# An attention output laid out as 96r + 32k + p instead of 3p + k, in a kernel of linear attention and two feed-forward stages

## The chip, the cores and the metric

The kernel runs on one core of one Trainium2 chip. The metric is the device time of one execution in microseconds, as the median of several runs. The profile shows one execution of its own. All arithmetic that matters here is float32 on TensorE, where one product of float32 operands appears in the trace as two MATMUL instructions (called passes below), each with its own LDWEIGHTS.

## The reference

```python
for t in range(S):                       # B, H, S, D = 4, 8, 768, 48
    state = f[:, :, t, :, None] * state + einsum('bhd,bhe->bhde', k[:, :, t], v[:, :, t])
    y[:, :, t] = einsum('bhd,bhde->bhe', q[:, :, t], state)      # f = sigmoid(f_logit)
x = y.transpose(0, 2, 1, 3).reshape(B * S, H * D)                # 3072 x 384
h = x @ w_in                                                     # 384 x 2048
x = (h * sigmoid(1.702 * h)) @ w_out                             # 2048 x 384
p = domain_probs / (domain_probs.sum(-1) + 1e-9)                 # 4 experts
out = sum over e of p[:, e] * (relu(x @ w1[e]) @ w2[e])          # w1: 384 x 1024
```

## The kernel before

The work falls into eight halves of a batch entry (384 tokens each: `HALVES`), each in three chunks (`CH`) of 128 tokens. The eight heads are held as four pairs (`PAIRS`), the two heads of a pair in the two 64-partition halves. Attention of a chunk is a masked score matrix (built level by level, `level`), its product with v, plus the product of the running state with q.

The program has four stretches. First the attention of half 0 alone (0 to 60 us). Then, seven times over, the attention of half n beside the first feed-forward of half n-1 (60 to 540 us): `both` goes through 18 slots, and in each slot TensorE does `hidden` (nine matmuls of 384 columns with w_in for one block of 128 hidden units), then the attention steps that the table `plan` puts there, then `layer_out` (nine matmuls with w_out, two slots behind). Then the first feed-forward of half 7, then the experts up to the end. I call the attention halves beside a feed-forward half 1 to half 7.

The attention output of chunk c is step `y`. In `plan`, y of chunk 0 (y0) stands in slot 13, y1 in slot 15, y2 in slot 16, each followed by step `update` of the state where one is wanted: TensorE multiplies v with k (L1781), VectorE adds the result to the faded state (L1406). y2 needs the state of update 1: its first matmul already waits for it, since it writes the PSUM bank that update 1 is read from.

From half 1 on, `y_columns` writes y straight in the layout that w_in wants: features on partitions, tokens on columns, as three tiles m of 128 features. A column tile of TensorE (32 output rows, `tile_position=(0, 32r)`) belongs to pair r. Feature dm stands in tile m at partition p with dm = 3p + m, so the 32 rows of pair r in tile m are every third of its 96 features: 16 of the one head, 16 of the other. For each m there are therefore two products of v a pair, one a head, over the columns that `v_columns` cuts with a stride of three. v is kept with 48 zero columns between the two heads of a pair, so that the rows of the other head get zeros added:

```python
    VW = 3 * D
    ...
    def v_columns(c, h, m):
        lo = h % 2 * D + m
        return v_sb[:, c, h // 2, lo:lo + 31 * KT + 1:KT]
```

That makes 3 x 2 x 4 = 24 products of v a chunk (32 rows by 128 columns), and then 3 x 4 = 12 products of the state where there is one (all chunks but chunk 0 of a first half). Consecutive products go to the four column tiles in turn.

In half 0 (`fine(n)`) y has tokens on partitions. VectorE adds the diagonal part into `y_rows` (L1395), TensorE turns that by three transposes over `y_rows[:, m::KT]` (L1790), ScalarE and VectorE write `x_h` and `x_l` (L1073, L1418).

Around these steps, ScalarE does the sigmoid of slot j (`gelu_sigmoid`, L1083), VectorE the product (L1425), ScalarE the rounded high part `g_h` (L1090), GpSimd the low part `g_l` (L836), and `layer_out` of block j waits for `g_l` of block j. In slot 15 VectorE also turns the gates of the next half (`next_turn`, L1234) ahead of the state update of chunk 1, GpSimd then computes the next decays (L717). In slots 11 and 12 VectorE copies the bands of the score matrix (L1343). SyncE issues nearly all loads, in program order.

Of the kernel before, what the change touches and what calls it, by code (L numbers as in the profile page):

```python
# [19 lines left out]
ALU = mybir.AluOpType  # L20
# [3 lines left out]
P = 128  # L24
# [4 lines left out]
def moe_of_attention_kernel(nc: bass.Bass, q, k, v, f_logit, w_in, w_out, probs, w1, w2, out, x2_dram):  # L29
    B, H, S, D = q.shape  # L30
    TOK = B * S
    DM = H * D
# [103 lines left out]
    VW = 3 * D  # L136
# [131 lines left out]
    win_v = w_in.rearrange("(p k) n -> k p n", p=P)  # L268
# [30 lines left out]
    def v_heads(c):  # L299

        return v_sb[:, c, :, :].rearrange("p r (x d) -> p r x d", x=3)[:, :, 0::2, :]

    def v_head(c, h):
        lo = h % 2 * 2 * D
        return v_sb[:, c, h // 2, lo:lo + D]

    def v_columns(c, h, m):
        lo = h % 2 * D + m
        return v_sb[:, c, h // 2, lo:lo + 31 * KT + 1:KT]

    def state_columns(r, m):

        return state[:, r, m::KT]
# [90 lines left out]
    with ExitStack() as ctx:  # L404
# [84 lines left out]
        def _(sp):  # L489
# [53 lines left out]
            def load_v(b, a, n):  # L543

                sp.wait_ge(unit_ready, n * UNITS)
                for c in range(CH):
                    for j in range(2):
                        sp.dma_start(v_sb[:, c, :, 2 * j * D:(2 * j + 1) * D],
                                     v_v[b, a, c, :, j::2, :]).then_inc(v_loaded, 16)
# [6 lines left out]
            def load_piece(i):  # L556
# [6 lines left out]
                src = win_v[o // FF, :, o % FF:o % FF + width] if which == "in" else wout_v[:, o // DM, :]  # L563
# [7 lines left out]
            for c in range(CH):  # L571
                for j in range(2):
                    sp.dma_start(v_sb[:, c, :, 2 * j * D:(2 * j + 1) * D],
                                 v_v[0, 0, c, :, j::2, :]).then_inc(v_loaded, 16)
# [645 lines left out]
        def _(dve):  # L1220
# [4 lines left out]
            dve.memset(v_sb[:, :, :, D:2 * D], 0.0).then_inc(zeros_ready, 1)  # L1225

            def step(s, c, n, a, b):
# [162 lines left out]
                if s == "y" and fine(n):  # L1390
# [4 lines left out]
                    dve.tensor_tensor(y_rows[:, :], ring[u % 3][:, 0:DM], v_diag[:, :], ALU.add)\  # L1395
# [165 lines left out]
        def _(pe):  # L1561
# [67 lines left out]
            def y_columns(c, n, a):  # L1629
# [8 lines left out]
                for m in range(KT):  # L1638
                    for j in range(2):
                        for r in range(PAIRS):  # L1640
                            last = add(r, m, v_columns(c, 2 * r + j, m), scores_T[:, c, 2 * r + j, :],
                                       m == 0 and j == 0, m == KT - 1 and j == 1 and not from_state)
# [10 lines left out]
            def step(s, c, n, a, b):  # L1653
# [130 lines left out]
                if s == "x" and fine(n):  # L1784
# [4 lines left out]
                    for m in range(KT):  # L1789
                        last = pe.transpose(ring[u % 3][:, m * P:(m + 1) * P], y_rows[:, m::KT], ident[:, :])  # L1790
# [158 lines left out]
```

## Time and profile before

| | us |
|---|---|
| median of 3 runs | 1356.08 |
| lowest, highest | 1355.3, 1356.3 |
| the profiled execution | 1355.08 |
| its span | 1353.3 |
| TensorE busy | 1326.8 (98%) |
| VectorE busy | 890.9 (66%) |
| ScalarE busy | 568.4 (42%) |
| GpSimd busy | 629.0 (46%) |

The span runs from the first to the last instruction in the trace, the execution's time is 1.78 us longer. The granted clock of TensorE is 0.999 over the span. A row of a timeline gives the start and the length of a run of like instructions, the engine, the line in the kernel, what is written from what, and in brackets how long the engine was idle ahead of it and what ended that. The end of a matmul is modelled (start to result), so that consecutive matmuls overlap in the rows, and the distance from start to start tells their pace.

### The profile page before, as it was taken

To read this page: it belongs to the slowest core of one execution; us is meant where nothing else is said; L and a number is where in the kernel's file an instruction comes from. 1 tells how busy PE (TensorE), PEld (TensorE's weight loads), DVE (VectorE), ACT (ScalarE), POOL (GpSimd) and SP (SyncE) were. 2 spreads that over 40 slices of the span, in tenths; PEclk is the share of its full clock that TensorE was granted. 3 is DMA by queue.
4 is the path that set the end of the run, shared out by engine and by line. 5 is a ranking of instruction groups with operands and counts; after the bars stand their busy time and mean duration, and the time that the engine had idled before them with its cause. 6 is when DMAs were issued, how large, how long until landed. Compare 5 with 4: busy or idle time off the path is not lost.

```text
span 1353.3 us, 26477 instructions
## 1 busy us (share of the span) xinstructions
PE 1326.8 (98%) x10837; PEld 1233.1 (91%) x10837; DVE 890.9 (66%) x1354; ACT 568.4 (42%) x975; POOL 629.0 (46%) x721
## 2 busy tenths in 40 slices
PE   6899999999999999999999999999999999999999
PEld 5788999999999999998999999999999999999998
DVE  8786858475858583566666666666666666666666
ACT  5673636363636363453233333333323433334341
POOL 8786747484747573655121212112212544443330
PEclk9999999999999999999999999999999999999999
DMA  9636252525252521220101101010001112222211
GB/s 157 135 74 104 60 84 63 86 61 85 62 88 59 87 59 40 79 74 24 35 13 35 36 13 35 12 36 24 25 24 59 36 47 70 71 70 75 66 35 47
DMA packets 240200, 79.34 MB, mean 59 GB/s; under 512 B 189136, under 2 KB 238544, under 8 KB 240080
## 3 DMA queue, kind: packets, MB, share of 16 engines
q1 hardware_dynamic: 201680, 74.11, 23.0%
q10 hardware_dynamic: 38400, 3.55, 2.2%
q8 instruction: 85, 1.39, 0.4%
q14 instruction: 35, 0.29, 0.1%
HBM read 67.83 MB, written 9.78 MB: 57 GB/s over the span
## 4 chain that ended last, share of the span: by engine, by line
PE 89%; ACT 3%; DVE 2%; issue 2%; POOL 2%; SPq 1%; DMA 1%; ACTq 0%; DVEq 0%; POOLq 0%
PE bank L1917 10%; PE bank L1915 10%; PE bank L1916 10%; PE bank L1851 9%; PE bank L1852 9%; PE bank L1850 9%; PE bank L1823 5%; PE bank L1582 4%; PE bank L1825 4%; PE bank L1824 4%; PE bank L1580 4%; PE bank L1581 4%; PE bank L1635 3%; PE bank L1591 1%; PE bank L1781 1%
## 5 line engine op out<-in xcount | busy, mean ns | idle before, releaser
L1529 DVE SCALAR_TENSOR_TENSOR acc<-bank,p_n,acc 128x384 f32<-128x384 f32 x384 | 235.0, 612 | 67.9 <-PE bank L1917 62.9
L1917 PE MATMUL bank<-w_h,h_l 128*128 128x384 f32 x768 | 257.3, 335 | 0.0
L1915 PE MATMUL bank<-w_h,h_h 128*128 128x384 f32 x768 | 257.2, 335 | 0.0
L1916 PE MATMUL bank<-w_l,h_h 128*128 128x384 f32 x768 | 257.0, 335 | 0.0
L1513 DVE TENSOR_TENSOR bank<-bank,x_copy 128x512 f32<-128x512 f32 x192 | 124.5, 694 | 165.9 <-ACT x_copy L1187 102.4
L836 POOL TENSOR_TENSOR g_l<-sig,g_h 128x384 fp32r<-128x384 f32 x128 | 157.7, 1232 | 157.4 <-ACT g_h L1090 157.3
L1852 PE MATMUL bank<-xs,we_l 128*128 128x512 f32 x528 | 206.5, 391 | 0.0
L1851 PE MATMUL bank<-xs,we_h 128*128 128x512 f32 x528 | 206.4, 391 | 0.0
L1850 PE MATMUL bank<-xs,we_h 128*128 128x512 f32 x528 | 205.5, 389 | 0.7 <-issue 0.7
L888 POOL TENSOR_TENSOR we_l<-we_raw,we_h 128x384 fp32r<-128x384 f32 x96 | 96.5, 1033 | 215.4 <-ACT we_h L1155 215.3
L1187 ACT ACTIVATE x_copy<-bank 128x512 f32<-128x512 f32 x144 | 86.1, 598 | 222.1 <-PE bank L1852 221.7
L1519 DVE SCALAR_TENSOR_TENSOR h_l<-bank,h_h 128x512 fp32r<-128x512 f32 x192 | 130.5, 681 | 31.9 <-ACT h_h L1181 31.9
L1181 ACT ACTIVATE h_h<-bank 128x512 fp32r<-128x512 f32 x192 | 114.7, 598 | 79.9 <-DVE bank L1513 79.8
L1915 PEld LDWEIGHTS bank<-w_h,h_h 128*128 128x128 f32 x768 | 144.3, 188 | 1.8
L1916 PEld LDWEIGHTS bank<-w_l,h_h 128*128 128x128 f32 x768 | 144.2, 188 | 1.8
L1425 DVE TENSOR_TENSOR sig<-bank,sig 128x384 f32<-128x384 f32 x128 | 70.4, 553 | 113.8 <-ACT sig L1083 113.0
L899 POOL TENSOR_TENSOR w_l<-w_raw,w_h 128x384 fp32r<-128x384 f32 x64 | 64.2, 1023 | 173.3 <-ACT w_h L1163 173.3
L1917 PEld LDWEIGHTS bank<-w_h,h_l 128*128 128x128 f32 x768 | 144.2, 188 | 0.0
L1823 PE MATMUL bank<-g_h,wout_h 128*128 128x384 f32 x384 | 136.6, 356 | 0.9 <-POOL g_l L836 0.9
L1580 PE MATMUL bank<-x_h,win_h 128*128 128x384 f32 x384 | 128.6, 335 | 2.3 <-DVE x_l L1418 1.3
L1824 PE MATMUL bank<-g_l,wout_h 128*128 128x384 f32 x384 | 128.9, 336 | 0.0
L1825 PE MATMUL bank<-g_h,wout_l 128*128 128x384 f32 x384 | 128.9, 336 | 0.0
(156 smaller groups left out, 2387.2 us busy)
## 6 DMA issues: line engine op xcount, KB each, us to landing
we_raw<-in_moe_w SPq DMA_DIRECT2D x32, 384.0 KB, 3.9
w_raw<-in_moe_w SPq DMA_DIRECT2D x32, 384.0 KB, 3.3
v_sb<-in_v SPq DMA_DIRECT2D x48, 96.0 KB, 2.7
x_dram<-work SPq DMA_DIRECT2D x8, 576.0 KB, 4.7
x_raw<-x_dram SPq DMA_DIRECT2D x12, 384.0 KB, 4.4
f_raw<-in_f_logit SPq DMA_DIRECT2D x56, 72.0 KB, 2.1
q_raw<-in_q SPq DMA_DIRECT2D x56, 72.0 KB, 2.0
k_raw<-in_k SPq DMA_DIRECT2D x56, 72.0 KB, 2.1
```

Of the source, the lines that this page charges most:

```text
L836: pool.tensor_tensor(g_l[:, j % RING, :], sig[:, j % 2, :], g_h[:, j % RING, :].bitcast(F32), ALU.subtract).then_inc(gl_ready, 1)
L1529: dve.scalar_tensor_tensor(acc[:, pr * TT + i, :], y_bank[y % 3][:, 0:DM], p_n[:, col:col + 1], acc[:, pr * TT + i, :], ALU.mult, ALU.add) ...
L1580: pe.matmul(dst, lh, rh, start=i == 0, stop=False)
L1823: pe.matmul(dst, wh, gh, start=j == 0, stop=False)
L1824: pe.matmul(dst, wh, gl, start=False, stop=False)
L1825: last = pe.matmul(dst, wl, gh, start=False, stop=j == FT - 1)
L1850: pe.matmul(dst[:, :], lh, rh, start=start, stop=False, skip_group_check=True)
L1851: pe.matmul(dst[:, :], lh, rl, start=False, stop=False, skip_group_check=True)
L1852: return pe.matmul(dst[:, :], ll, rh, start=False, stop=True, skip_group_check=True)
L1915: pe.matmul(dst, hh, wh, start=f == 0, stop=False)
L1916: pe.matmul(dst, hh, wl, start=False, stop=False)
L1917: last = pe.matmul(dst, hl, wh, start=False, stop=f == 1)
```

## The change: another order of the features

Feature dm now stands in tile k at partition 32r + p with dm = 96r + 32k + p. The 32 rows of pair r in tile k are 32 consecutive features of its 96: of tile 0 all belong to the first head, of tile 1 sixteen to each head, of tile 2 all to the second head. A list `TILE_PARTS` names the four parts (tile, head of the pair, first column of v); the v products of a chunk are 4 parts x 4 pairs = 16. Between the two heads v now has 16 zero columns, and the row of a pair is 128 wide instead of 144. w_in is loaded with its rows in the same order, in the same twelve pieces. In half 0 the addition into `y_rows` writes the features tile by tile, so that the transposes read 128 consecutive columns.

```diff
-    VW = 3 * D
+    VW = 2 * GAP
...
-    win_v = w_in.rearrange("(p k) n -> k p n", p=P)
+    win_v = w_in.rearrange("(r k p) n -> k r p n", r=PAIRS, k=KT)
...
-    def v_columns(c, h, m):
-        lo = h % 2 * D + m
-        return v_sb[:, c, h // 2, lo:lo + 31 * KT + 1:KT]
+
+    TILE_PARTS = [(0, 0, 0), (1, 0, SQ), (1, 1, D), (2, 1, D + SQ)]
+
+    def v_columns(c, r, first):
+
+        return v_sb[:, c, r, first:first + SQ]
 
     def state_columns(r, m):
 
-        return state[:, r, m::KT]
+        return state[:, r, m * SQ:(m + 1) * SQ]
...
-                        sp.dma_start(v_sb[:, c, :, 2 * j * D:(2 * j + 1) * D],
+                        sp.dma_start(v_sb[:, c, :, j * GAP:j * GAP + D],
...
-            dve.memset(v_sb[:, :, :, D:2 * D], 0.0).then_inc(zeros_ready, 1)
+            dve.memset(v_sb[:, :, :, D:GAP], 0.0).then_inc(zeros_ready, 1)
...
-                    dve.tensor_tensor(y_rows[:, :], ring[u % 3][:, 0:DM], v_diag[:, :], ALU.add)\
+                    by_tile = y_rows[:, :].rearrange("p (k r x) -> p r k x", k=KT, r=PAIRS)
+                    dve.tensor_tensor(by_tile, ring[u % 3][:, 0:DM].rearrange("p (r k x) -> p r k x", k=KT, r=PAIRS),
+                                      v_diag[:, :].rearrange("p (r k x) -> p r k x", k=KT, r=PAIRS), ALU.add)\
...
-                for m in range(KT):
-                    for j in range(2):
-                        for r in range(PAIRS):
-                            last = add(r, m, v_columns(c, 2 * r + j, m), scores_T[:, c, 2 * r + j, :],
-                                       m == 0 and j == 0, m == KT - 1 and j == 1 and not from_state)
+                for m, j, first in TILE_PARTS:
+                    for r in range(PAIRS):
+                        last = add(r, m, v_columns(c, r, first), scores_T[:, c, 2 * r + j, :],
+                                   m == 0, m == KT - 1 and not from_state)
...
-                        last = pe.transpose(ring[u % 3][:, m * P:(m + 1) * P], y_rows[:, m::KT], ident[:, :])
+                        last = pe.transpose(ring[u % 3][:, m * P:(m + 1) * P], y_rows[:, m * P:(m + 1) * P], ident[:, :])
```

TensorE around y1 of half 1, before (the last three numbers of a row are the shape and the count of products, each of which is two passes):

```order
L1582 MATMUL bank<-x_h_71,win_l 128x384
L1635 MATMUL bank<-scores_T,v_sb 32x128 x24
L1635 MATMUL bank<-q_T,state 32x128 x12
L1781 MATMUL bank<-v_sb,k_rows 112x96 x4
L1823 MATMUL bank<-g_h,wout_h 128x384
```

The same place, after:

```order
L1588 MATMUL bank<-x_h_71,win_l 128x384
L1641 MATMUL bank<-scores_T,v_sb 32x128 x16
L1641 MATMUL bank<-q_T,state 32x128 x12
L1786 MATMUL bank<-v_sb,k_rows 112x96 x4
L1828 MATMUL bank<-g_h,wout_h 128x384
```

Eight v products are gone, and all that stands ahead and behind is what it was. The same holds at each of the 21 chunks of halves 1 to 7.

VectorE at the end of half 0, from the turn of the gates of half 1 to the low part of x of chunk 0, before:

```order
L1234 STREAM_TRANSPOSE gate_T<-f_raw 128x1536
L1289 TENSOR_REDUCE diag<-diag_prod 128x8 x3
L1395 TENSOR_TENSOR y_rows<-bank,v_diag 128x384
L1406 TENSOR_TENSOR state<-bank,state_faded 48x4x48 x2
L1436 TENSOR_TENSOR wout_l<-work,wout_h 128x384
L1418 TENSOR_TENSOR x_l_72<-bank,x_h_71 128x3x128
```

And after:

```order
L1238 STREAM_TRANSPOSE gate_T<-f_raw 128x1536
L1293 TENSOR_REDUCE diag<-diag_prod 128x8 x3
L1400 TENSOR_TENSOR y_rows<-bank,v_diag 128x4x3x32
L1412 TENSOR_TENSOR state<-bank,state_faded 48x4x48 x2
L1442 TENSOR_TENSOR wout_l<-work,wout_h 128x384
L1424 TENSOR_TENSOR x_l_72<-bank,x_h_71 128x3x128
```

No instruction moves; the addition goes over runs of 32 instead of one run of 384.

## Rows read from the trace of the kernel before

**Rows 1.** The page: busy time of TensorE, and the chain that ended last.

```profile
PE 1326.8 (98%) x10837; PEld 1233.1 (91%) x10837; DVE 890.9 (66%) x1354; ACT 568.4 (42%) x975; POOL 629.0 (46%) x721
PE 89%; ACT 3%; DVE 2%; issue 2%; POOL 2%; SPq 1%; DMA 1%; ACTq 0%; DVEq 0%; POOLq 0%
```

**Rows 2.** Groups of TensorE by shape: count of passes, busy us, mean ns, idle.

```profile
L1635 PE MATMUL bank<-scores_T,v_sb 128*32 128x128 f32 x1008 | 32.3, 276 | 1.4 <-DVE state L1406 1.2 <-issue 0.2
L1635 PE MATMUL bank<-q_T,state 128*32 128x128 f32 x432 | 15.1, 273 | 0.0
```

**Rows 3.** Timeline of TensorE, y0 of half 1.

```profile
110.76 1.54 PE L1635 MATMUL bank<-scores_T,v_sb 128*32 128x128 f32 x48
112.11 0.84 PE L1635 MATMUL bank<-q_T,state 128*32 128x128 f32 x24
```

**Rows 4.** Timeline of the weight loads, windows cut inside y1 (halves 5, 3).

```profile
392.92 0.58 PEld L1635 LDWEIGHTS bank<-scores_T,v_sb 128*32 128x32 f32 x20
...
257.89 0.26 PEld L1635 LDWEIGHTS bank<-scores_T,v_sb 128*32 128x32 f32 x8
```

**Rows 5.** Timeline of TensorE in half 1: levels 4 and 5 of the scores.

```profile
84.05 1.02 PE L1591 MATMUL bank<-q_split,k_T 128*16 128x32 f32 x96
...
88.92 1.53 PE L1591 MATMUL bank<-q_split,k_T 128*32 128x64 f32 x48 [0.49 <-POOL k_T L773]
```

**Rows 6.** Timelines, y2 in halves 2 and 5: VectorE's state update, then TensorE.

```profile
191.85 0.72 DVE L1406 TENSOR_TENSOR state<-bank,state_faded 48x192 f32<-48x192 f32 x2
...
193.75 1.54 PE L1635 MATMUL bank<-scores_T,v_sb 128*32 128x128 f32 x48
...
395.47 0.68 DVE L1406 TENSOR_TENSOR state<-bank,state_faded 48x192 f32<-48x192 f32 x2
...
396.92 1.54 PE L1635 MATMUL bank<-scores_T,v_sb 128*32 128x128 f32 x48
```

**Rows 7.** Timelines of half 1 from slot 12 to its end, all engines.

```profile
106.31 9.04 SPq L512 DMA_DIRECT2D f_raw<-in_f_logit  x16
...
118.86 0.53 ACT L968 ACTIVATE wout_h<-work 128x384 fp32r<-128x384 f32 x1 [4.28 <-DMA work<-in_moe_w_out]
...
123.88 1.77 DVE L1234 STREAM_TRANSPOSE gate_T<-f_raw 128x1536 f32<-128x1536 f32 x1
...
126.31 1.54 PE L1635 MATMUL bank<-scores_T,v_sb 128*32 128x128 f32 x48 [0.95 <-DVE state L1406]
...
129.62 1.01 POOL L836 TENSOR_TENSOR g_l<-sig,g_h 128x384 fp32r<-128x384 f32 x1
...
130.68 0.44 PE L1823 MATMUL bank<-g_h,wout_h 128*128 128x384 f32 x1 [0.42 <-POOL g_l L836]
```

**Rows 8.** Timelines of half 3, y2 and the last block of w_out.

```profile
261.88 1.54 PE L1635 MATMUL bank<-scores_T,v_sb 128*32 128x128 f32 x48 [0.24 <-DVE state L1406]
...
264.21 1.01 POOL L836 TENSOR_TENSOR g_l<-sig,g_h 128x384 fp32r<-128x384 f32 x1
...
265.66 0.33 PE L1823 MATMUL bank<-g_h,wout_h 128*128 128x384 f32 x1
```

**Rows 9.** Timelines of half 6, slot 13: GpSimd's low part, then TensorE.

```profile
447.41 3.97 POOL L836 TENSOR_TENSOR g_l<-sig,g_h 128x384 fp32r<-128x384 f32 x1 [1.31 <-ACT g_h L1090]
...
451.71 0.42 PE L1823 MATMUL bank<-g_h,wout_h 128*128 128x384 f32 x1
```

**Rows 10.** Timeline of VectorE in half 0.

```profile
5.91 0.54 DVE L1225 MEMSET v_sb<- 128x576 f32 x1
9.62 3.22 DVE L1255 TENSOR_TENSOR q_T<-q_T,gate_T 128x512 f32<-128x512 f32 x3 [3.17 <-ACT q_T L997]
...
53.13 0.56 DVE L1395 TENSOR_TENSOR y_rows<-bank,v_diag 128x384 f32<-128x384 f32 x1 [0.63 <-PE bank L1771]
...
56.00 0.56 DVE L1418 TENSOR_TENSOR x_l<-bank,x_h 128x384 fp32r<-128x384 f32 x1
```

**Rows 11.** The page: DMA issues of w_in's late pieces, KB each, us to landing.

```profile
stage<-in_moe_w_in SPq DMA_DIRECT2D x6, 256.0 KB, 4.1
```

**Rows 12.** The stretch 25 to 45 us: busy by engine, granted clock.

```profile
25.00:45.00 20.00, 15.25 (x111) 14.03 (x112) 18.67 (x28) 17.36 (x39) 15.65 (x19) 0.91 0.64 108
```

More of the change, by code:

```diff
@@ L299, in v_heads @@
     def v_heads(c):
-        return v_sb[:, c, :, :].rearrange("p r (x d) -> p r x d", x=3)[:, :, 0::2, :]
+        return v_sb[:, c, :, :].rearrange("p r (j x) -> p r j x", j=2)[:, :, :, 0:D]
     def v_head(c, h):
-        lo = h % 2 * 2 * D
+        lo = h % 2 * GAP
         return v_sb[:, c, h // 2, lo:lo + D]
-    def v_columns(c, h, m):
-        lo = h % 2 * D + m
-        return v_sb[:, c, h // 2, lo:lo + 31 * KT + 1:KT]
+    TILE_PARTS = [(0, 0, 0), (1, 0, SQ), (1, 1, D), (2, 1, D + SQ)]
+    def v_columns(c, r, first):
+        return v_sb[:, c, r, first:first + SQ]
     def state_columns(r, m):
-        return state[:, r, m::KT]
+        return state[:, r, m * SQ:(m + 1) * SQ]
     def scores_of(i, L, n):
@@ L562, in load_piece @@
                 dst = stages[stage_of[i]][:, 0:width]
-                src = win_v[o // FF, :, o % FF:o % FF + width] if which == "in" else wout_v[:, o // DM, :]
+                src = win_v[o // FF, :, :, o % FF:o % FF + width] if which == "in" else wout_v[:, o // DM, :]
                 sp.dma_start(dst, src).then_inc(w_loaded[stage_of[i]], 16)
@@ L572, in _ @@
                 for j in range(2):
-                    sp.dma_start(v_sb[:, c, :, 2 * j * D:(2 * j + 1) * D],
+                    sp.dma_start(v_sb[:, c, :, j * GAP:j * GAP + D],
                                  v_v[0, 0, c, :, j::2, :]).then_inc(v_loaded, 16)
```

## The prediction

> **What bounds the kernel now.** I read the page first: TensorE is busy 98% of the span and makes up 89% of the chain that ended last [rows 1]. So an instruction that TensorE loses is worth its time unless something else is late behind it, and the question is only how much of it comes back as a wait. Next the groups by shape: the products of v in y are 1008 passes, those of the state 432 [rows 2]. 1008 is 21 chunks x 24 products x 2 passes, so it is halves 1 to 7 alone. Their mean of 276 ns is start to result and says nothing on pace, since they overlap; pace comes from the timeline. Last I looked, around each y in each of the seven halves, at what TensorE waits for and by how much the other engines are ahead of it: that is where a saving can get lost.
>
> **What the removed products cost.** In y0 of half 1 the 48 passes of v take 1.35 us up to the first pass of the state (112.11 - 110.76) [rows 3], that is 28 ns each with the start-up. Inside the stream it is cleaner: a window that catches 20 passes shows 0.58 us of weight loads, one that catches 8 shows 0.26 [rows 4], so 12 passes take 0.32 us. The passes go round the four column tiles, so 12 passes are three rounds, and a round is 0.107 us. With the start-up it is 1.35 / 12 = 0.1125. I take 0.109 us a round, between the two and nearer to the stream. What sets the round? The levels of the scores use the same kind of tiles with fewer moving columns. Level 4 has 96 passes of 32 columns over four tiles: 24 rounds in about 1.02 - 0.20 us, 0.034 us a round. Level 5 has 48 passes of 64 columns over two tiles: 24 rounds in about 1.53 - 0.22 us, 0.055 us a round [rows 5]. With 128 columns it is 0.109. Time goes with the moving columns (0.034, 0.055, 0.109), so a tile is bound by streaming 128 columns of scores, two clocks each at 2.4 GHz plus a little, and not by a fixed price of an instruction. A pass that goes away takes its share of a round with it.
>
> Before, a chunk has 48 passes of v, 12 rounds. After, it has 32, 8 rounds. Saved are 4 x 0.109 = 0.437 us a chunk, and over 21 chunks **9.18 us**. The order within the rounds stays (four pairs in turn), so no tile gets two passes in a row. The state products keep their count.
>
> The Trainium skill, page "TensorE: Matmul & The Clock Gate", section "Wait — 56ns, not 53.3ns?", says that the start-to-start distance of matmuls never drops below some 25 ns, however few the columns. The 27 ns a pass seen here would sit right on that floor. By the page the saving would be an estimated 21 x 16 x 25 ns = 8.4 us. The trace of this kernel speaks against a floor of that height: level 4 runs its passes 8.5 ns apart.
>
> **What else changes.** The weights of y are now 32 consecutive columns instead of every third. The loads run beside the streaming of the other tiles, and level 5 turns the same 32 weight columns, consecutive ones, round in 0.055 us, half a round of y [rows 5]; if the strided loads were hidden, consecutive ones bring nothing. I take 0. Were they what sets the round, there would be a gain on top (a rival, below).
>
> The addition into `y_rows` took 0.56 us over one run of 384; the low part of x, the same count of elements over three runs of 128, took 0.56 as well [rows 10]. Runs of 32 I have no row for. From below nothing (a reading in runs costs nothing from 384 to 128), from above, say, half as much again, 0.28 us, three times on the chain of half 0, 0.84 us. I take 0.1 us in all, near the lower end since the nearest row shows no cost. The memset of v's gap shrinks from 576 to 192 elements a partition, but VectorE then idles 3.17 us for ScalarE [rows 10]: nothing. The transposes of `y_rows` with consecutive columns: nothing, same count. Loading v writes runs of the same 192 bytes: nothing. w_in's pieces have the same bytes and the same whole rows, from four blocks of 32 rows; a landing of 4.1 us [rows 11] may move by some tenths either way, with more than that between landing and first use in nearly every piece. I take 0 and keep -0.3 to +1 us for the range.
>
> **What the halves give back.** TensorE comes to each wait 0.437 us earlier a chunk passed, and the cover of the waits decides.
>
> Half 1 gives nothing. ScalarE stands at 118.86 for a piece of w_out [rows 7], which SyncE issued behind sixteen other loads that began at 106.31, ahead of y0 at 110.76. Behind it in ScalarE's order stand the sigmoid of the gates and of slot 15, then VectorE's turn of the gates at 123.88, the state update, and y2 waits for that, 0.95 us already [rows 7]. All of it is fixed by the load, not by TensorE. So what y0 and y1 save comes back as a longer wait ahead of y2: 0.95 + 0.87 = 1.8 us. And what y2 saves is lost too, because the last block of w_out waits for GpSimd's low part, done at 129.62 + 1.01 = 130.63, and TensorE waits for it 0.42 us already [rows 7]. Lost: 3 x 0.437 = **1.31 us**.
>
> Half 3: y2 waits 0.24 us for the state behind the gates' turn [rows 8], so what y1 saves is lost, **0.44**. The turn follows work that y0's end starts, so y0's gain stays. After y2, GpSimd's part is done at 265.22 and TensorE wants it at 265.66 [rows 8]; 0.44 less leaves it at 265.22, and a signal takes some 0.05 (130.63 to 130.68 in half 1). Lost: **0.05**.
>
> Half 6: GpSimd's low part of slot 11 ends at 447.41 + 3.97 = 451.38, TensorE comes at 451.71 [rows 9]. It will come at 451.27 and wait to 451.43. Lost: **0.16**.
>
> The others have cover. In half 2 the state is done at 192.57 and y2 starts at 193.75, 1.18 us later, likewise in halves 4 and 6; in half 5 it is 396.15 against 396.92, 0.77 us [rows 6]. Both are more than the 0.44 that y1 takes from them. Half 7 has no turn of the gates ahead of the state.
>
> **The sum.** 9.18 - 1.31 - 0.44 - 0.05 - 0.16 - 0.1 = 7.1 us. The profiled execution has a span of 1353.3 and a time of 1355.08, 1.78 more. Its span would become 1346.2, its time 1348.0. The median of the runs, 1356.08, lies 1.0 above that execution, so the median after is 1356.08 - 7.1 = **1349.0 us**.
>
> **The rivals.**
> A, all of it arrives: the chains that I take as fixed move along with TensorE (the late load of w_out in half 1 above all), or the lost tenths are made up. Then 9.2 us, 1346.9. For it speaks that many chains start from TensorE's own work; against it that SyncE's row of half 1 starts ahead of y0 [rows 7].
> B, the weight loads set the round. The Trainium skill, page "SBUF — State Buffer", section "Door 1: The DMA port swizzle", says that each access that crosses to a new 16-byte line pays; with a stride of three floats most do, and no run so far shows what it costs here. As a mechanism of this kernel: if 0.109 is the time of a strided load and consecutive columns take the round down by a tenth (to 0.098), v and state products go from 18 rounds to 14 shorter ones. That is 18 x 0.109 - 14 x 0.098 = 0.59 us a full chunk, some 12 us over 21 chunks, less about 2.5 given back: 1346.5. Against it: the rounds scale with the moving columns [rows 5].
> C, the other engines take more. I measured cover from one execution; DMA landings move by tenths, and the shares of VectorE and GpSimd between slots 13 and 17 are dense. If all odd halves lose what half 1 loses (four times 1.31) and the even ones 0.3 each, 9.2 - 5.2 - 0.9 - 0.1 = 3 us remain: 1353.1.
> D, slower. In half 0 TensorE waits between small bursts and its clock falls: over 25 to 45 us the granted clock is 0.91 [rows 12], so 1.8 us of full clock are lost in one dip. If the longer wait ahead of y2 made the clock fall once a half, that would cost seven times 1.8 = 12.6 us against 9.2 saved: +3.4 us, 1359.5. It decides from six dips on. Against it: half 1 already waits 0.95 us there, and over the span the clock is 0.999, with no dip outside half 0.
>
> **Chances.** My forecast (6.4 to 7.8 us) 0.60, A 0.15, B 0.06, C and what lies between it and the forecast 0.16, D and the like 0.03. The range goes from B's and A's times to short of C, 1346.2 to 1352.8. What a measurement can tell from no change is about 0.2%, 2.7 us: faster than 1353.4 I give 0.91, within it 0.06, slower 0.03.
>
> **What the profile after would show.** 672 passes of v instead of 1008, with the start of the state products 0.92 us after that of v instead of 1.35. TensorE's busy time lower by about 9. In half 1 a wait of 1.8 us ahead of y2 and one of about 0.85 at the last block of w_out; in half 3 a wait of 0.7 ahead of y2; in half 6 one of about 0.15 in slot 13. Wrong I would be if the distance stayed near 1.2 (a price by instruction or by weight columns), or if new waits showed in halves 2, 4, 5 or 7.

## The result, and the profile after

The changed kernel takes 1365.47 us (median of 4 runs, 1363.56 to 1365.97), the kernel before 1356.19 in the same sessions (4 runs). The ratio is 1.0064 with a 95% interval of 1.0048 to 1.008. It is slower by 9 us, where I forecast 7 us faster. None of the rivals had it; to slower than the kernel before I had given a chance of 0.03.

The profiled execution has a span of 1363.5 us, its time is 1365.28. The page of the kernel after, its busy line and the chain of work that ended last, answering to [rows 1], and from the groups of TensorE by shape the products of v and of the state, answering to [rows 2]:

```profile
PE 1320.8 (97%) x10501; PEld 1226.4 (90%) x10501; DVE 886.8 (65%) x1354; ACT 567.9 (42%) x975; POOL 631.3 (46%) x721
...
PE 88%; SPq 4%; ACT 3%; POOL 2%; issue 2%; DVE 1%; DMA 1%; ACTq 0%; DVEq 0%; POOLq 0%
```

```profile
L1641 PE MATMUL bank<-scores_T,v_sb 128*32 128x128 f32 x672 | 22.7, 276 | 1.2 <-DVE state L1412 1.2
L1641 PE MATMUL bank<-q_T,state 128*32 128x128 f32 x432 | 15.1, 273 | 0.0
```

TensorE runs 336 passes fewer and is busy 6.0 us less, yet the span is 10.2 us longer. In the chain SPq, the queue in which SyncE issues the loads, went from 1% to 4%: by these rounded shares some 40 us more of it are issues of loads. That points away from y.

To find the place I cut both spans at the first `hidden` product of each stretch (read from the timelines of TensorE). "Half 0" is the attention alone, "half 1" to "half 7" the attention beside a feed-forward, "the rest" the last feed-forward and the experts.

| us | half 0 | half 1 | halves 2 to 7 | the rest |
|---|---|---|---|---|
| before | 60.2 | 72.2 | 404.5 | 816.4 |
| after | 73.2 | 75.7 | 397.5 | 817.2 |
| difference | +13.0 | +3.5 | -7.0 | +0.8 |

So the gain came where I had put it, and two stretches in which I had put the change of the load at nothing (half 0 and half 1) took back more than twice as much.

**Half 0.** The timeline of SyncE's queue, after; a row is a run of like DMA issues, and its length is how long SyncE was at it:

```profile
9.56 2.29 SPq L568 DMA_DIRECT2D work<-in_moe_w_in  x3
11.89 5.90 SPq L568 DMA_DIRECT2D stage<-in_moe_w_in  x3
17.83 2.42 SPq L568 DMA_DIRECT2D stage<-in_moe_w_out  x1
20.30 10.48 SPq L577 DMA_DIRECT2D v_sb<-in_v  x6
30.82 1.74 SPq L579 DMA_DIRECT2D p_raw<-in_moe_domain_probs  x1
32.61 9.69 SPq L516 DMA_DIRECT2D f_raw<-in_f_logit  x16
```

The same rows of before:

```profile
11.84 1.38 SPq L564 DMA_DIRECT2D stage<-in_moe_w_in  x3
13.26 0.43 SPq L564 DMA_DIRECT2D stage<-in_moe_w_out  x1
13.74 5.01 SPq L573 DMA_DIRECT2D v_sb<-in_v  x6
...
19.34 10.06 SPq L512 DMA_DIRECT2D f_raw<-in_f_logit  x16
```

The first three pieces of w_in are issued as fast as before. The next three take 5.90 us instead of 1.38, the six loads of v 10.48 instead of 5.01, and the gates' loads start at 32.61 instead of 19.34. The profile shows no wait of SyncE for a semaphore there; each issue takes longer. The view of DMA over 9 to 32 us points to the reason: one digit for each of 40 slices, the busy share of the 16 DMA engines in tenths, and below it the rate. After, then before:

```profile
DMA  9999994222222222222248922222742256265479
GB/s 164 161 165 162 164 153 65 78 100 93 100 107 100 100 103 100 103 100 100 107 132 266 245 77 89 100 107 100 182 128 100 103 148 162 98 160 123 93 156 181
```

```profile
DMA  9999999999999999999947954746547376666459
GB/s 164 164 163 163 164 181 204 324 395 388 381 374 374 391 312 259 232 171 169 100 17 23 35 70 53 98 47 86 54 66 85 52 99 66 78 79 77 58 94 329
```

While the pieces of w_in move, the DMA engines are busy for 9 tenths or more before, at up to 395 GB/s. After, they stand at 2 tenths and about 100 GB/s from 13 to 20 us and again behind that: a quarter of the engines at a quarter of the rate. The source pattern of a piece is now (r, p, n), four blocks of 32 rows; it was (p, n), 128 rows. My reading is that a pattern whose outermost count is 4 is carried by 4 of the 16 engines (the experiments below test it). This is what the Trainium skill states on the page "DMA: Bandwidth & Descriptors", section "Why a DMA increments its semaphore by 16 and not by 1", under "How many engines (k)": k is the largest number up to 16 that divides the slowest dimension of both patterns. Its "Rules for kernel authors" put it as advice: "Put a dim whose size is a multiple of 16 (ideally the 128 partitions) outermost". By that rule the trace agrees, with 2 tenths and 100 GB/s.

What followed on ScalarE and TensorE (timelines, after; in brackets the idle time ahead of a row and what ended it), and the stretch of 25 to 45 us, answering to [rows 12]:

```profile
43.84 1.48 ACT L1017 ACTIVATE f_raw<-f_raw 128x1536 f32<-128x1536 f32 x1 [12.56 <-DMA f_raw<-in_f_logit]
```

```profile
46.17 6.94 PE L1733 MATMUL bank<-q_split,k_T 128*128 128x128 f32 x48 [13.91 <-ACT q_split L1048]
```

```profile
25.00:45.00 20.00, 6.36 (x40) 5.88 (x40) 9.52 (x15) 5.55 (x11) 7.62 (x9) 0.67 0.59 102
```

The sigmoid of half 1's gates stands in ScalarE's order ahead of work of half 0. It finds its load 12.6 us late, and TensorE idles 13.9 us behind it. Its granted clock is also lower over the stretch of 25 to 45 us: 0.67 after, 0.91 before (a mean of the two levels, 1.0 for 2.4 GHz and 0.5 for 1.2 GHz).

**Half 1.** Four of the six late pieces of w_in stand in SyncE's order just ahead of the gates for half 2. Those gates' loads in SyncE's queue, before and after:

```profile
58.27 5.42 SPq L525 DMA_DIRECT2D f_raw<-in_f_logit  x8
```

```profile
71.57 4.96 SPq L529 DMA_DIRECT2D f_raw<-in_f_logit  x8
```

Here SyncE isn't late: it begins 1.9 us ahead of half 1 before (58.27 against 60.2) and 1.6 us ahead of it after (71.57 against 73.2), and it has issued all eight by 76.53. It is the landing that is late. The timelines of ScalarE and of TensorE, after:

```profile
84.03 1.17 ACT L1022 ACTIVATE f_raw<-f_raw 128x1152 f32<-128x1152 f32 x1 [4.29 <-DMA f_raw<-in_f_logit]
```

```profile
89.67 0.47 PE L1828 MATMUL bank<-g_h,wout_h 128*128 128x384 f32 x1 [1.74 <-POOL g_l L840]
```

ScalarE gets the gates only at 84.03, 7.5 us after the last of them was issued. Before, it waits for no DMA between 60 and 118 us.

**y itself.** Timelines of TensorE around three y, after: half 3's y2 (answering to [rows 8] and, for the distances, to [rows 3]), half 1's y2 and last block of w_out [rows 7], half 6's slot 13 [rows 9]:

```profile
262.55 1.08 PE L1641 MATMUL bank<-scores_T,v_sb 128*32 128x128 f32 x32
263.44 0.84 PE L1641 MATMUL bank<-q_T,state 128*32 128x128 f32 x24
...
142.81 1.08 PE L1641 MATMUL bank<-scores_T,v_sb 128*32 128x128 f32 x32 [1.23 <-DVE state L1412]
...
147.16 0.44 PE L1828 MATMUL bank<-g_h,wout_h 128*128 128x384 f32 x1 [0.86 <-POOL g_l L840]
...
463.45 0.45 PE L1828 MATMUL bank<-g_h,wout_h 128*128 128x384 f32 x1 [0.54 <-POOL g_l L840]
```

From the first pass of v to the first of the state it is 0.89 us for 32 passes, where it was 1.35 for 48. I had said 0.92. I had also said that TensorE's busy time would be lower by about 9 us. It is lower by 6.0 here and by 7.8 in run e1 below (1319.0 us), where the clock was low for a shorter time.

**The rest.** The +0.8 us sit at one place, the second block of the experts. TensorE's first pass of it, before and after:

```profile
611.94 0.47 PE L1850 MATMUL bank<-xs,we_h 128*128 128x512 f32 x1 [0.65 <-issue]
```

```profile
622.17 0.47 PE L1855 MATMUL bank<-xs,we_h 128*128 128x512 f32 x1 [1.41 <-issue]
```

It follows the end of GpSimd's part of `xs`, and GpSimd had waited for the last loads of x from DRAM. Its rows, before and after:

```profile
602.95 0.74 POOL L906 TENSOR_TENSOR x_raw<-x_raw 128x256 f32<-128x256 f32 x1 [4.69 <-DMA x_raw<-x_dram]
```

```profile
613.74 0.74 POOL L910 TENSOR_TENSOR x_raw<-x_raw 128x256 f32<-128x256 f32 x1 [6.01 <-DMA x_raw<-x_dram]
```

Neither x nor these loads are touched by the edit. I come back to this in the last experiment.

### The profile page after: what moved, and what is told of

Same layout as the page of the kernel before. It is cut to its first block, busy times and chain, and to the rows that moved or that the text cites. A ratio compares the mean times of both kernels' runs of the same rounds, so it can differ in the third digit from the quotient of the medians.

```text
span 1363.5 us, 25805 instructions
## 1 busy us (share of the span) xinstructions
PE 1320.8 (97%) x10501; PEld 1226.4 (90%) x10501; DVE 886.8 (65%) x1354; ACT 567.9 (42%) x975; POOL 631.3 (46%) x721
## 4 chain that ended last, share of the span: by engine, by line
PE 88%; SPq 4%; ACT 3%; POOL 2%; issue 2%; DVE 1%; DMA 1%; ACTq 0%; DVEq 0%; POOLq 0%
PE bank L1922 10%; PE bank L1920 10%; PE bank L1921 10%; PE bank L1856 9%; PE bank L1857 9%; PE bank L1855 9%; PE bank L1828 5%; PE bank L1830 4%; PE bank L1829 4%; PE bank L1588 4%; PE bank L1586 4%; PE bank L1587 4%; PE bank L1641 2%; PE bank L1597 1%; POOL g_l L840 1%
## 5 line engine op out<-in xcount | busy, mean ns | idle before, releaser
L1535 DVE SCALAR_TENSOR_TENSOR acc<-bank,p_n,acc 128x384 f32<-128x384 f32 x384 | 235.5, 613 | 67.8 <-PE bank L1922 62.9
```

The lines of the kernel that those rows point to most:

```text
L1535: dve.scalar_tensor_tensor(acc[:, pr * TT + i, :], y_bank[y % 3][:, 0:DM], p_n[:, col:col + 1], acc[:, pr * TT + i, :], ALU.mult, ALU.add) ...
```

## The experiments

The labels e1, e2 and so on name the runs. Each ratio is against the kernel before in the same session.

**The theories.** 1: w_in's pieces ride on as many DMA engines as the outermost count of their source gives, four here; all of half 0's and half 1's loss is that. 2: the loss has to do with y (v's narrower rows, `y_rows`, the products). 3: it is the blocks as such, their scattered rows in DRAM, whatever their number.

### The load undone, and the load alone

```diff
 # after, with the old source
-    win_v = w_in.rearrange("(r k p) n -> k r p n", r=PAIRS, k=KT)
+    win_v = w_in.rearrange("(p k) n -> k p n", p=P)
...
```

> The changed kernel with w_in loaded in the old row order (p k): rows of w_in then don't match the features, so the output is another one; nothing else differs. Theory 1 (the source of the w_in pieces, now four blocks of 32 rows with the blocks outermost, is carried by few DMA engines, so each piece lands late and SyncE's queue backs up): with the old source the stall of half 0 is gone, half 0 ends near 60.2 us as before, halves 1 to 7 give what the prediction said, and the time is 1349 us (1348 to 1350.5). Theory 2 (the slow part is the y side: the addition into y_rows, or v's new place): the stall stays, 1363 to 1366 us.

Measured (e1): 1350.11 us (1347.89 to 1351.6, 4 runs), ratio 0.995 with an interval of 0.9932 to 0.9967, against 1356.89. Half 0 ends at 61.6, half 1 lasts 72.0. Half 0 is 1.4 us longer than in the profiled execution of the kernel before (60.2), where I had expected no difference. The granted clock over 25 to 45 us was 0.83 here and 0.91 there, an estimated 20 x 0.08 = 1.6 us of full clock, which is enough for it. The clock of this stretch differs between executions, so half 0 of two kernels is only to be compared at the same clock.

The opposite edit, the new source in the kernel before:

```diff
 # before, with the new source
-    win_v = w_in.rearrange("(p k) n -> k p n", p=P)
+    win_v = w_in.rearrange("(r k p) n -> k r p n", r=PAIRS, k=KT)
...
```

> The kernel before with only the w_in load changed to the four-block source (output another one, as rows and features don't match). Theory 1: half 0 ends near 73.2 us instead of 60.2 and half 1 is 3 to 4 us longer, so 1372 to 1374 us. Theory 2: no change, 1356 us.

Measured (e2): 1372.37 us (1371.72 to 1372.46), ratio 1.0115 (1.01 to 1.013). Half 0 ends at 73.5, half 1 lasts 75.5.

What follows: the source of w_in alone makes the whole loss, with or without the new y. It costs 15 to 16 us (1365.47 against 1350.11, 1372.37 against 1356.89), and what is left of the change is worth 6.8 us. Theory 2 falls.

### The number of blocks

Sixteen blocks of 8 rows, then eight of 16, in place of four of 32:

```diff
-    win_v = w_in.rearrange("(r k p) n -> k r p n", r=PAIRS, k=KT)
+    win_v = w_in.rearrange("(r k p) n -> k r p n", r=16, k=KT)
```

> The changed kernel with the same form of source for w_in but 16 blocks of 8 rows outermost instead of 4 blocks of 32 (rows 24a + 8k + p; output another one). Theory 1: sixteen outermost blocks spread over sixteen DMA engines, pieces land as fast as before, 1349 us (1348 to 1350.5). Rival (theory 3): a source in blocks, which does not merge into one run of rows, is slow as such; then sixteen blocks are as slow or slower, 1363 us or more.

> The changed kernel with eight blocks of 16 rows outermost in the source of w_in (output another one). Theory 1 (the number of outermost blocks is the number of DMA engines that carry a piece): a piece lands in about twice the time of sixteen blocks and half that of four, and the end of half 0 lies between 62 and 73 us; time 1350 to 1358 us. If any number below sixteen were as bad as four: 1364 us.

Measured with 16 (e3): 1351.84 us (1349.8 to 1353.67), ratio 0.9961 (0.9947 to 0.9975), half 0 ends at 62.9. With 8 (e5): 1354.15 (1352.29 to 1356.6, 10 runs), ratio 0.9985 (0.9976 to 0.9994), half 0 ends at 69.8. With 4 it was 73.2, with 128 rows (the old source) 61.6.

The stretches of 14 to 15 us, in which by the order of the issues hardly anything but w_in moves, and of 15 to 18 us (the last two numbers of a row: busy share of the 16 DMA engines, which can come out somewhat above 1, and GB/s); first 16 blocks, then 8, then the kernel after with 4:

```profile
14.00:15.00 1.00, 1.00 1.06 301
15.00:18.00 3.00, 1.00 1.06 292
```

```profile
14.00:15.00 1.00, 1.00 0.53 157
15.00:18.00 3.00, 1.00 0.75 178
```

```profile
14.00:15.00 1.00, 1.00 0.26 98
15.00:18.00 3.00, 1.00 0.26 102
```

Over 14 to 15 us the share is 1.06, 0.53 and 0.26 for 16, 8 and 4 blocks: all, half and a quarter of the engines. (With 128 rows outermost it is 1.06 as well, in the kernel before.) The rate falls with it: 301, 157, 98 GB/s there, 292, 178, 102 over 15 to 18 us, where with 8 blocks other loads have joined in. With 16 blocks, more scattered than four, nearly all is back, so theory 3 falls and theory 1 holds. The 16 blocks are somewhat slower than the old source (292 against 343 GB/s over 15 to 18 us in e1). SyncE begins the gates' loads 1.2 us later (20.71 against 19.47) and half 0 ends 1.3 us later at the same clock of 0.83 over 25 to 45 us, and the time is 1.3 us above my range. These are single profiled executions, so I take it as a small loss of the blocks that is likely but not shown.

### Which pieces cost what

The first six pieces by the old source, the last six by the new:

```diff
+    old_v = w_in.rearrange("(p k) n -> k p n", p=P)
...
+                if i < 6:
+                    src = old_v[o // FF, :, o % FF:o % FF + width]
```

> The changed kernel with the first six pieces of w_in in the old row order and the last six by the new four-block source (output another one). By theory 1 the stall of half 0 is made by the first six alone: half 0 ends near 60 to 61.5 us. The last six are issued at 52 to 75 us into a queue that isn't behind, so what they cost shows alone: half 1 lasts 72 to 75.5 us. Time 1350 to 1353 us. If the late pieces make the stall: 1364 us.

Measured (e7): 1352.68 us (1351.85 to 1353.68), half 0 ends at 61.6, half 1 lasts 75.7, the later ones as in the kernel after, all as expected. So the late pieces make the 3.5 us of half 1 and the early ones the rest. [rows 11], which I had read as the late pieces, is the group of the six that go through `stage`: the three early ones of 11.84 us and three late ones. The timeline of ScalarE has the same wait as the kernel after:

```profile
72.75 1.17 ACT L1025 ACTIVATE f_raw<-f_raw 128x1152 f32<-128x1152 f32 x1 [4.62 <-DMA f_raw<-in_f_logit]
```

### The new order with a wide load

The new order of rows needs a source that falls into four blocks. But it can be cut the other way: one DMA for each block, with its 32 partitions outermost and all three tiles in it. That is four DMAs for three pieces, 16 for w_in instead of 12, into three stages side by side:

```diff
-    win_v = w_in.rearrange("(r k p) n -> k r p n", r=PAIRS, k=KT)
+    win_v = w_in.rearrange("(r k p) n -> r p k n", r=PAIRS, k=KT)
...
+                    for r in range(PAIRS):
+                        dst = t[r * SQ:(r + 1) * SQ, at_stage * WP:(at_stage + 3) * WP].rearrange("p (k n) -> p k n", k=KT)
+                        sp.dma_start(dst, win_v[r, :, :, o:o + WP]).then_inc(w_loaded[stage_of[i]], 16)
```

> The changed kernel, complete and with its own order of features, with w_in loaded by one DMA for each pair r and block of 512 columns: 32 rows outermost, all three tiles k at once into three stages that lie side by side; 16 DMAs instead of 12, each with 32 rows outermost. Stages of the late pieces are assigned anew so that three neighbours are free together. Theory 1: the stall of half 0 is gone but for some 1 us more of issue on SyncE, 1349 to 1351 us, below both kernels. Theory 3 (several dimensions in the source are slow): 1360 us or more.

Measured (e4): 1363.96 us (1363.53 to 1364.93), a miss by 13 us. Half 0 ends at 64.8, but half 1 lasts 82.6. The loads keep all DMA engines busy (share 1.08 over 15 to 18 us, at 226 GB/s, where the old source had 343); what is late is the queue. The timeline of SyncE's queue:

```profile
53.26 7.69 SPq L592 DMA_DIRECT2D x_stages<-in_moe_w_out  x3
61.07 1.78 SPq L586 DMA_DIRECT2D work<-in_moe_w_in  x4
72.01 0.35 SPq L592 DMA_DIRECT2D x_stages<-in_moe_w_out  x1
72.40 2.79 SPq L542 DMA_DIRECT2D f_raw<-in_f_logit  x6
```

A load of three pieces needs three stages at once, and with my assignment SyncE stood up to 9 us at a stage that was not yet read, ahead of the gates' loads, which came at 72.4 us instead of 58.3 in the kernel before. As in half 0 of the kernel after, the gates' loads are issued late, here for another cause. (In half 1 of the kernel after they were issued in time and landed late.)

So I gave the pieces other stages, put no load ahead of the gates that has to wait, and issued v and the probabilities behind the gates' blocks; and, as the control, the same with v in its old place:

```diff
 # against the run with wide loads (e4)
-    stage_of = [i % STAGES for i in range(14)] + [3, 0, 1, 2, 3, 4, 5, 6, 3, 4, 5, 0, 1, 2]
+    stage_of = [i % STAGES for i in range(14)] + [3, 0, 1, 2, 3, 4, 5, 6, 1, 2, 3, 0, 1, 2]
...
+            for i in (0, 3, 6):
+                load_piece(i)
+            if not V_LATE:
+                load_first_v()
+            for t, then in (("f", (7, 8, 9)), ("q", (10, 11)), ("k", (12, 13, 15, 14))):
+                load_blocks(t, 0, 1, 1)
+                if t == "f" and V_LATE:
+                    load_first_v()
+                for i in then:
+                    load_piece(i)
```

> The complete changed kernel with w_in in 16 wide loads (32 rows outermost, three tiles k at once), stages assigned so that SyncE never waits long for a free one, and the first loads of v and of the probabilities issued behind the blocks of the gates of half 1 instead of ahead of them. Theory 1 says the wide loads are fast and that e4 lost its time to SyncE's order: half 0 ends by 61 us, half 1 lasts 72, and the time is 1348 to 1350 us. If wide loads are slow by themselves: 1354 us or more.

> As the run with wide loads and late v, but v and the probabilities are loaded where they were, ahead of the gates' blocks. SyncE reaches the last block of the gates some 4 us later than in the kernel before (it did in e4), so half 0 ends near 64.5 us as in e4, and half 1 lasts 72 instead of e4's 82.6 us: 1352 to 1354 us.

Measured: with v late (e6) 1350.47 us (1348.88 to 1353.81), ratio 0.9957 (0.9944 to 0.9969), half 0 ends at 62.8, not by 61 as I had expected, half 1 lasts 71.1, and the time is 0.5 us above my range. With v early (e9) 1353.86 (1350.69 to 1358.94, 10 runs), ratio 0.9983 (0.9972 to 0.9994), half 0 ends at 64.9. Both beat the kernel before. What was left over in half 0 stands in ScalarE's timeline (v late):

```profile
17.48 0.63 ACT L1000 ACTIVATE win_h<-work 128x512 fp32r<-128x512 f32 x1 [2.95 <-DMA work<-in_moe_w_in]
```

A wide load has its first piece only when all three are there. So the first one was cut in two, piece 0 alone and then pieces 1 and 2:

```diff
+    WIDE = {0: 1, 1: 2, 3: 3, 15: 3, 19: 3}
...
-            for i in (0, 3, 6):
+            for i in (0, 1, 3, 6):
```

> The wide loads with v behind the gates' blocks, and the first wide load cut in two: four transfers of 32 rows for piece 0 alone, then four for pieces 1 and 2 together. ScalarE's first copy of w_in should wait under 1 us for a DMA (2.9 us with one wide load for three pieces), so that half 0 ends at about 61 to 62 us (62.8 with the uncut load), half 1 lasts 71 to 72 us and each later half as before: 1348 to 1350 us. If the 1.2 us that the uncut version loses in half 0 come from elsewhere (v landing late, the queue), half 0 still ends at 62.5 to 63.5 and the time is 1349.5 to 1351.

> The wide loads with v behind the gates' blocks once more, on the chip of the other two, to compare the cut first load with: 1349.5 to 1351.5 us (1350.47 at first), half 0 ends at 62.5 to 63.5 us.

> The kernel before with one edit: the loads of the first v and of the probabilities are issued behind the blocks of the gates of half 1. If the gain of the wide loads with v late over those with v early (3.4 us) came from the place of v only because the queue was behind there, it is worth nothing here, where the gates' blocks are not waited for: 1355.5 to 1357 us. If v's place were worth something by itself, this kernel would take under 1354 us; if v now lands too late for its first readers, over 1358.

Measured, all three on one chip: cut (e10) 1349.15 us (1347.79 to 1355.67), ratio 0.9951 (0.9932 to 0.9969), half 0 ends at 60.7, half 1 lasts 72.0, and ScalarE waits for no DMA between 9 and 60 us. Uncut (e12) 1349.94 (1349.38 to 1351.13), ratio 0.995 (0.9938 to 0.9962), half 0 ends at 62.8, and ScalarE has its wait for w_in again (2.92 us). The cut takes that wait away. Of the 2.0 us between the two halves 0, though, an estimated 1.6 are clock: over 25 to 45 us it is 0.91 with the cut and 0.83 without, and 0.08 of 20 us is 1.6. So what the cut is worth in the time is not shown. The kernel before with v late (e11): 1356.98 (1354.66 to 1360.02, 12 runs), ratio 1.0002 (0.9991 to 1.0012). So v's place is worth nothing by itself; it was worth 3.4 us only where the queue ahead of the gates had become long.

### The +0.8 us at the experts

Every kernel with 672 passes of v had it, however w_in was loaded (the rest 817.0 to 817.4 us in ten of them), no kernel with 1008 passes (816.4 to 816.5 in three). In the window of the last loads of x the page of DMA has, in those ten and not in those three, a transfer that is no data:

```profile
q8 instruction: 1, 0.02, 0.8%
```

This queue brings instructions, 85 transfers over the span before, 83 after, so with 672 instructions of TensorE fewer (336 passes and their weight loads) two blocks fewer. The last of these loads ends in another way, too. Share of the DMA engines and rate in the 0.8 us that end 0.1 us before it lands, in the kernel before and in the kernel after:

```profile
601.98:602.78 0.80, 1.00 1.09 387
```

```profile
612.77:613.57 0.80, 1.00 0.08 28
```

In the four kernels without such a transfer (the fourth is the test below) the share is 1.08 to 1.10, in the ten with it 0.07 to 0.18. A sixteenth is 0.06, so in most of the ten about a single one of the 16 DMA engines is still at work (0.07 or 0.08 in seven), and the load is complete only with it.

My reading: TensorE's code comes in blocks (85 of them bring 1.39 MB, 16 KB each), a block is fetched as the engine gets to it, and with code taken out ahead of it that moment shifts against the work. To test it I moved it by about half a block in the other direction: 30 products of one column on TensorE in half 0, 120 instructions.

```diff
+                            if r < 2:
+                                pe.matmul(ring[u % 3][:, r * P:r * P + 1], k_T[:, x * P:(x + 1) * P],
+                                          q_split[:, x, 0, 0:1], start=True, stop=True)
```

> The kernel with the cut first wide load, and 30 products of one moving column more on TensorE in half 0 (60 passes and their weight loads, 120 instructions; each writes a column that the next product writes again). They are there to move the blocks in which TensorE's instructions are fetched against the work, not for what they compute. Theory: in all ten kernels with 672 passes one fetch of instructions falls among the last loads of x for the experts and makes them land 1 to 1.5 us later, which TensorE pays with 0.6 to 0.9 us at the second block of the experts; in the three with 1008 passes none falls there. 120 instructions earlier is about half a block, some 10 us of TensorE's work here, so no fetch should lie among these loads: GpSimd's wait for x_raw goes from 5.8 to 4.5 to 4.8 us, TensorE's from 1.2 to 0.5 to 0.7, and the stretch from the last attention half to the end from 817.1 to 816.3 to 816.5 us. If the later landing comes from something else (x's other order, the place of the buffers), GpSimd still waits 5.7 to 6.3 us and the stretch stays at 817.0 to 817.3. The time as a whole: half 0 gets 1 to 5 us longer by the added passes, so 1349.5 to 1353.5 us under either.

Measured (e13): GpSimd's wait, and the products' group on the page (its wait stands behind the bar):

```profile
614.18 0.74 POOL L938 TENSOR_TENSOR x_raw<-x_raw 128x256 f32<-128x256 f32 x1 [4.40 <-DMA x_raw<-x_dram]
```

```profile
L1887 PE MATMUL bank<-xs,we_h 128*128 128x512 f32 x528 | 205.4, 389 | 0.7 <-issue 0.7
```

4.40 us instead of 5.81, 0.7 instead of 1.2, the rest 816.6 instead of 817.1, and no fetch in the window (they stand at 595 and 625 us). The tail of the load is gone as well:

```profile
613.21:614.01 0.80, 1.00 1.09 382
```

The rise of the wait is gone as expected (GpSimd's is even 0.1 us shorter than I had said). That one fetch of 0.02 MB delays loads of 384 KB by over a microsecond rests on this coincidence in fourteen kernels, one of them made for the test. That the engine which finishes late is the one that carried the fetch fits, but is not shown.

The time as a whole was a miss: 1360.8 us, where I said 1349.5 to 1353.5. But the ten executions fall into two groups, and the median lies between them. Five took 1350.7 to 1355.7 us at a mean granted clock of 0.995 to 0.998, near what I said; five took 1365.9 to 1370.9 at 0.980 to 0.986. The profiled execution is one of the second group (1366.6 us), and half 0 ends at 78.1 us in it. TensorE is busy nearly all the time there, at half clock:

```profile
45.00:60.00 15.00, 14.82 (x70) 14.53 (x69) 7.38 (x11) 7.10 (x17) 6.07 (x9) 0.50 0.44 73
```

The granted clock is 0.50, that is 1.2 GHz, over a stretch of products of one column between short bursts of 128. Without them (e10) the same stretch has 1.00. In both the clock falls near 30 us, after 5 us in which TensorE did little (busy 1.80 of 5 us here, 0.69 in e10). In e10 it is back at 1.00 over 35 to 40 us, here over 70 to 75. A pair of the added passes takes 0.15 us at the full clock (30.33 to 30.48) and 0.28 at half (44.26 to 44.54), so my 1 to 5 us for all 60 was right at the full clock, and I had not priced what the clock can do beside them. No execution of the other kernels has a mean clock under 0.991, so the long low stretch goes with the added passes; what decides from one execution to the next whether it comes is not shown.

## Why the prediction was wrong

**The step that failed** is the one on w_in: "same bytes and whole rows, from four blocks of 32 rows ... may move by some tenths either way ... I take 0". It measured 17 us in the spans (e2 against the kernel before: 13.3 in half 0, 3.3 in half 1) and 15.5 in the medians (1372.37 against 1356.89). Three things went wrong in one sentence. I looked at what a row of the source is and not at how the pattern is nested. I took the landing of 4.1 us in [rows 11] for that of the six late pieces, while it is the median of three early and three late ones, and I did not look at the early ones' place in the queue, ahead of the gates' loads that half 0 waits for. And I bounded the cost by the slack between landing and first use of w_in itself, when the cost falls on what is queued behind: w_in was in time, the gates were not. ScalarE's 12.56 us are a wait for f_raw.

**What held**, read in e1, where the loads are the old ones. The saving in rounds: 0.46 us a chunk less between v and state (1.35 to 0.89, in e1 as in the kernel after), forecast 0.437. Halves 2 to 7 gained 7.0 us (after) and 7.1 (e1), forecast 18 x 0.437 - 0.65 = 7.2. Half 1 gained 0.2 us (e1), forecast nothing, since its chain hangs on a late load: the wait at the last block of w_out is 0.86 us in e1 as in the kernel after, forecast 0.85. The wait ahead of y2, forecast 1.8, is 1.51 in e1, with another new one of 0.28 some 13 us ahead of it, for GpSimd's `g_l`; it is 1.23 in the kernel after, where half 1 runs behind another delay. The addition into `y_rows` takes 0.56 us in runs of 32 as well, so nothing instead of 0.1.

**What the sum got right by cancelling.** Half 6 lost more than its 0.16: the wait is 0.54 us. GpSimd's low part there runs beside VectorE's copies of the bands and takes 3.97 us [rows 9], where one without them takes 1.01 [rows 8]. My reading: the copies start when a DMA lands and not when TensorE is done, so an earlier TensorE finds them later in its own time (at 458.71, with ScalarE's sigmoid at 457.86; before at 446.65, with the sigmoid at 446.42). It changes with the execution: in e1 half 6 has no such wait, and halves 2 and 4 have one (0.24 and 0.49 us), where I had seen cover, because I had looked at y2 and not at slot 13. Half 3 lost nothing where I had given up 0.49 (it gained 1.6 us). That the halves together came within 0.2 us of the forecast is in part luck: these misses cancel.

**What the sum lacked**: 0.8 us at the experts, by the reading above from TensorE's shorter code.

**The rivals.** B, that the weight loads set the round, falls, though single weight loads did get shorter. The weight loads of v by shape, before (stride of three) and after (consecutive columns); the last number before the second bar is the mean of one in ns:

```profile
L1635 PEld LDWEIGHTS bank<-scores_T,v_sb 128*32 128x32 f32 x1008 | 26.9, 123 | 6.9 <-issue 4.5 <-DVE state L1406 1.8 <-DVE x_l L1418 0.5
```

```profile
L1641 PEld LDWEIGHTS bank<-scores_T,v_sb 128*32 128x32 f32 x672 | 17.1, 109 | 6.5 <-issue 4.7 <-DVE state L1412 1.5 <-DVE x_l L1424 0.3
```

A load is 14 ns shorter with consecutive columns. But inside the stream, away from its ends, the loads start 27.3 ns apart on average both before and after, a round of 0.109 us: the shorter load brings nothing.

A falls by half 1, C by halves 5 and 7, which gained 1.3 us and more each. D, the clock: in half 0 the clock is low, but beside the wait for the gates. In half 1 of the kernel after it is 0.86 over 84 to 96 us, behind waits of 1.5 and 1.7 us that come from the late gates as well. None appeared at the longer waits ahead of y2. The slower side of the forecast came by a mechanism that I had on the table as a term of the sum and not as a rival.

**The floor of 25 ns.** By the Trainium skill, page "TensorE: Matmul & The Clock Gate", section "Wait — 56ns, not 53.3ns?", matmuls never start less than some 25 ns apart. As weighed in the prediction, the saving by it would be an estimated 8.4 us raw. 32 passes in 0.89 us are 27.8 ns each with the start-up, 48 in 1.35 were 28.1, so y alone can't tell such a floor from a stream of 128 columns. Level 4 with its 8.5 ns [rows 5] speaks against the floor, in this stream over four column tiles.

**With its loads mended the change comes close to what I had forecast.** 1349.15 us (e10) against the forecast of 1349.0, the lowest median here, though the runs can't tell it from the uncut load's 1349.94. Some of the closeness is luck: e10 has loads that the forecast knew nothing of, and it pays the 0.8 us at the experts. The cleaner figure is e1, the change with the old loads: 6.8 us less than the kernel before, forecast 7.1.

## What to carry to other kernels

When a layout changes, read the nesting of every DMA pattern anew, not its bytes: an outermost count of 4 gives 4 of 16 DMA engines, and the cost lands on the loads queued behind it. Split such a load into several with a long outermost dimension, and issue nothing that waits for a buffer ahead of a load that something waits for. Loading the first piece alone took away a wait of 2.9 us on ScalarE, but no time that the runs can tell. Fewer instructions on TensorE also move where its code is fetched; a new wait of under a microsecond far from the edit can be that. And read the granted clock of a stretch before comparing its length between two profiles: 0.83 instead of 0.91 over 20 us is 1.6 us.

## What the runs showed of the hardware

- DMAs from DRAM with an outermost source count of 16, 8 and 4 moved 292, 178 and 102 GB/s over 15 to 18 us, with 128 rows 352 (343 in e1). The busy share of the 16 DMA engines over 14 to 15 us was 1.06, 0.53 and 0.26, with 128 rows 1.06.
- An issue by SyncE took 0.46 us (1.38 / 3) when all engines carried the loads ahead of it, and 2.0 (5.90 / 3) to 2.4 us (17.83, one load of w_out) when a quarter of them did, with no wait for a semaphore in the profile.
- Loads behind such a transfer can also be issued in time and land late: in half 1 of the kernel after, the gates' loads, all issued by 76.53 us, reached ScalarE at 84.03.
- One fetch of TensorE's code (0.02 MB) beside two loads of 384 KB went with a landing over 1 us later and a last 0.8 us in which 0.07 to 0.18 of the DMA engines were busy, in ten kernels of ten; without it the share was 1.08 to 1.10, in four of four.
- A weight load of 32 columns took 123 ns with a stride of 12 bytes and 109 with consecutive columns, at the same distance of 27.3 ns between starts.
- With 60 passes of one column among products of 128, five of ten executions ran at a mean clock of 0.980 to 0.986 and took 1365.9 to 1370.9 us, the other five at 0.995 to 0.998 and 1350.7 to 1355.7. In the profiled one the clock was 0.50 over 45 to 60 us with TensorE busy 99% of it, and half 0 was 17 us longer than in e10 (78.1 against 60.7).
